# Wider token units in a fused pooled-attention and two-layer MLP kernel: from six units (2 of 576, 4 of 720 tokens) to five (1 of 576, 4 of 864)

## What is computed

```
k_p, v_p = k, v averaged over groups of 8 rows        # 576 keys -> 72
scores = q @ k_p.T / sqrt(64); attn = softmax(scores)
x = attn @ v_p                                        # 8 batches x 8 heads x 576 rows x 64
x = x as 4608 tokens x 512
x = (s * relu(x @ w_in)**2 + b) @ w_out               # 512 -> 2048 -> 512
y = silu(x @ w2_in) @ w2_out                          # 512 -> 2048 -> 512
```

## Time and profile before

| | |
|---|---|
| median of 3 executions | 1635.66 us (1635.04 to 1637.19) |
| the profiled execution, its own time | 1636.79 us |
| span from first to last instruction of it | 1635.0 us |
| PE busy | 1589.4 us, 97% of the span |
| DVE, ACT, POOL busy | 1044.5, 902.2, 220.4 us |
| moved by DMA | 483.82 MB, mean 296 GB/s |
| instructions | 26389, of them 10582 matmuls |

### The profile page before, as it was taken

The page is one execution under the profiler, slowest core; times in us unless marked ns, Lnnn a source line. Parts: engine busy times, 40 slices in busy tenths (PEclk is TensorE's granted clock), DMA queues, the critical chain, the costliest instruction groups (busy, mean ns, idle before and its releaser), DMA issues.

```text
span 1635.0 us, 26389 instructions
## 1 busy us (share of the span) xinstructions
PE 1589.4 (97%) x10582; PEld 1577.5 (96%) x10582; DVE 1044.5 (64%) x1201; ACT 902.2 (55%) x1156; POOL 220.4 (13%) x294
## 2 busy tenths in 40 slices
PE   7999998999989999899999999999999999999998
PEld 7999998999989999899999999999999999999998
DVE  6687686576675765756656846756657657446455
ACT  4575664755536646467455467355476454473442
POOL 5220120122111222201102011011011010000000
PEclk8999999999999999999999999999999999999999
DMA  6799999998999988988888988888988888877886
GB/s 199 280 338 367 343 354 362 319 325 307 314 312 349 329 302 300 323 316 270 277 263 279 315 297 274 269 274 276 332 276 273 265 270 288 317 267 265 266 268 216
DMA packets 138008, 483.82 MB, mean 296 GB/s; under 512 B 14752, under 2 KB 14752, under 8 KB 135840
## 3 DMA queue, kind: packets, MB, share of 16 engines
q1 hardware_dynamic: 134080, 472.70, 84.2%
q10 hardware_dynamic: 3808, 9.44, 1.5%
HBM read 405.67 MB, written 76.41 MB: 295 GB/s over the span
## 4 chain that ended last, share of the span: by engine, by line
PE 85%; DVE 6%; DMA 4%; ACT 4%; issue 1%; SPq 0%; ACTq 0%; DVEq 0%
PE a_ps L802 21%; PE a_ps L824 19%; PE b_ps L802 15%; PE b_ps L824 14%; PE a_ps L728 3%; PE a_ps L752 3%; PE t_ps L695 2%; DMA xa_dram<-probs 2%; DMA ring<-w_dram 2%; PE t_ps L682 2%; PE t_ps L668 2%; PE t_ps L752 2%; PE b_ps L752 1%; PE b_ps L728 1%; DVE gq L1287 1%
## 5 line engine op out<-in xcount | busy, mean ns | idle before, releaser
L802 PE MATMUL a_ps<-xc_hi,ring 128*128 128x360 f32 (+1 forms) x1536 | 386.4, 320 | 6.7 <-DMA ring<-w_dram 3.8
L824 PE MATMUL a_ps<-sp_hi,ring 128*128 128x360 f32 (+1 forms) x1536 | 367.6, 317 | 5.6 <-DMA ring<-w_dram 5.6
L802 PE MATMUL b_ps<-xc_hi,ring 128*128 128x360 f32 (+1 forms) x1152 | 291.3, 319 | 3.6 <-DVE gq L1262 2.2
L802 PEld LDWEIGHTS a_ps<-xc_hi,ring 128*128 128x128 f32 x1536 | 269.9, 189 | 8.0 <-ACT gq L1019 4.0
L824 PE MATMUL b_ps<-sp_hi,ring 128*128 128x360 f32 (+1 forms) x1152 | 275.7, 317 | 0.0
L1303 DVE TENSOR_TENSOR sp_lo<-gq,sp_hi 128x1440 fp32r<-128x1440 f32 (+3 forms) x156 | 194.8, 1271 | 121.2 <-ACT sp_hi L997 121.1
L824 PEld LDWEIGHTS a_ps<-sp_hi,ring 128*128 128x128 f32 x1536 | 265.4, 188 | 6.0 <-issue 6.0
L802 PE MATMUL a_ps<-xc_lo,ring 128*128 128x360 f32 (+1 forms) x768 | 243.4, 317 | 0.0
L824 PE MATMUL a_ps<-sp_lo,ring 128*128 128x360 f32 (+1 forms) x768 | 242.7, 316 | 0.0
L802 PEld LDWEIGHTS b_ps<-xc_hi,ring 128*128 128x128 f32 x1152 | 202.4, 189 | 4.2 <-DVE gq L1262 2.7
L824 PEld LDWEIGHTS b_ps<-sp_hi,ring 128*128 128x128 f32 x1152 | 199.9, 189 | 0.0
(11 more groups left out here) (168 smaller groups left out, 2516.7 us busy)
## 6 DMA issues: line engine op xcount, KB each, us to landing
ring<-w_dram SPq DMA_DIRECT2D x672, 512.0 KB, 4.6
w_dram<-w_stage SPq DMA_DIRECT2D x32, 1024.0 KB, 5.8
w_dram<-ring SPq DMA_DIRECT2D x48, 512.0 KB, 5.5
w_raw<-weights SPq DMA_DIRECT2D x16, 1024.0 KB, 6.8
k_stage<-kT SPq DMA_DIRECT2D x30, 288.0 KB, 5.4
q_sb<-qT SPq DMA_DIRECT2D x30, 288.0 KB, 5.6
v_stage<-vP SPq DMA_DIRECT2D x30, 288.0 KB
xa_dram<-probs SPq DMA_DIRECT2D x28, 288.0 KB, 5.5
```

Source lines behind the costliest of these rows:

```text
L802: last = nc.tensor.matmul(bank[:, half, 0:th], w, xc_of(x, th)[:, j, k, :], start=(first and k == 0 and i == 0), stop=(k == 1 and i == 2), ...
L824: last = nc.tensor.matmul(bank[:, m, 0:th], w, split_of(g, th, turn, 2 * c + half), start=(first and half == 0 and i == 0), stop=(end and ...
```

## The change

Units: one of 576 tokens and four of 864, so `HALVES` = 288 and four times 432 columns, and ten phases instead of twelve. 560 granule loads instead of 672.

Places: `sp_hi` and `sp_lo` have 16*432 columns each; the unit of 288 columns makes six places of them, those of 432 columns four. Places no longer go round over the whole run: each phase starts with place 0, and the first operands of a phase wait for the last slot of the phase before (in phase 0: for the last stores out of `w_stage`, which now lies in the same columns).

Slots of `dhi`, `dlo` and `combine`: written in tables `HIGHS`, `LOWS` and `SUMS`, one for four and one for six places. The tables for four places hold the slots of the code before. With six places the operands (2,0) and (3,0) are made in slots 21 to 23 instead of 31 and 35, the second part of (1,0) in slot 18 instead of 22, (2,1) and (3,1) two and four slots earlier than before, (4,0) one earlier, (4,1) one later, the rest as before.

Attention: the first unit takes five jobs instead of four (the first of them from slot 2 instead of 0, the last in slots 92 to 100), the narrow unit seven instead of six, by a new table `SEVEN`; two wide units take six (a new `SIX`), one four (a new `FOUR`), the last none. The number of jobs is 28 as before.

Memory: `w_raw1`, which had a buffer of its own, is laid over `gq`; the program is built with `dynamic_dma_scratch_size=4096`.

```diff
-HALVES = (288,) * 2 + (360,) * 4
+HALVES = (288,) + (432,) * 4
-PIECES = tuple(2 if i < 4 else 1 for i in range(len(DOWN)))
-PIECE_END = tuple(sum(PIECES[:i + 1]) for i in range(len(DOWN)))
-SPLITS = PIECE_END[-1]
-LATE_COMBOS = {7: (4, 0), 9: (4, 1), 13: (6, 0), 17: (6, 1)}
+SPLITS = len(DOWN) + 4
+HIGHS = {
...
+    6: {8: [(0, 0, 0)], 15: [(0, 0, 1), (1, 0, 0)], 18: [(1, 0, 1)], 21: [(2, 0, 0)], 22: [(3, 0, 0), (0, 1, 0)],
+        27: [(0, 1, 1)], 29: [(1, 1, 0), (1, 1, 1)], 31: [(2, 1, 0)], 33: [(3, 1, 0)], 38: [(4, 0, 0)], 42: [(4, 1, 0)],
+        43: [(5, 0, 0)], 45: [(5, 1, 0)], 47: [(6, 0, 0)], 49: [(6, 1, 0)]},
+}
...
-PLACES = 4
+SPLIT_COLUMNS = 16 * TM
+PLACES = tuple(min(6, SPLIT_COLUMNS // (4 * th)) for th in HALVES)
...
-XC_FIRST, SP_FIRST, G_FIRST = 14 * HB, 4 * PLACES * HB, 2 * FS * HB
+XC_FIRST, SP_FIRST, G_FIRST = 14 * HB, 2 * FPIECES * HB, 2 * FS * HB
...
+def operand_order(ph):
+    return [(j, h) for j, h, part in in_order(HIGHS[PLACES[ph // 2]]) if part == 0]
+
+
+def place_of_operand(ph, j, h):
+
+    order, places = operand_order(ph), PLACES[ph // 2]
+    nth = order.index((j, h))
+    if nth < places:
+        return nth, gran(ph - 1, SLOTS - 1) if ph else None
+    return nth % places, gran(ph, SLOTS_UP + 2 * DOWN.index(order[nth - places]) + 1)
...
-FIRST_UP = 2
+FIRST_UP = (2, 3)
 FIRST_TURNS = (
...
+    (2, 2, 3, 4, 6, 8, 8, 11, 12, 13, 13, 15, 15),
+    (17, 21, 21, 22, 23, 26, 29, 31, 32, 34, 34, 36, 37),
+    (64, 64, 65, 67, 69, 70, 70, 71, 72, 73, 75, 75, 75),
+    (77, 78, 79, 80, 80, 84, 84, 86, 86, 87, 88, 88, 89),
+    (92, 92, 94, 94, 95, 97, 97, 98, 98, 99, 99, 100, 100),
 )
...
+SEVEN = (
+    (0, 0, 0, 0, 1, 2, 2, 4, 5, 6, 8, 8, 8),
+    (13, 14, 14, 14, 15, 18, 19, 20, 21, 22, 22, 24, 24),
+    (26, 27, 28, 29, 29, 31, 31, 33, 33, 36, 37, 37, 37),
+    (40, 40, 40, 42, 42, 44, 44, 47, 47, 49, 49, 50, 51),
+    (51, 52, 52, 55, 55, 58, 58, 59, 59, 60, 61, 62, 62),
+    (64, 65, 65, 66, 66, 68, 69, 71, 71, 74, 75, 76, 76),
+    (78, 79, 80, 81, 83, 84, 84, 86, 86, 88, 88, 91, 92),
+)
...
-UNIT_TURNS = (FIRST_TURNS, SIX, SIX, FOUR, FOUR, FOUR)
+UNIT_TURNS = (FIRST_TURNS, SEVEN, SIX, SIX, FOUR)
...
-        w_raw = [over("w_raw0", yb_at, 0, [4, 512]), sb("w_raw1", [P, 4, 512])]
+        w_raw = [over("w_raw0", yb_at, 0, [4, 512]), over("w_raw1", gq_at, G_FIRST + 2 * KC * HB, [4, 512])]
...
             def load_x(s):
                 if s:
-                    sp.wait_ge(dlo_ready, (2 * s - 1) * SPLITS + PIECE_END[7])
-                    sp.wait_ge(combined, (2 * s - 1) * len(COMBOS) + COMBOS.index((4, 1, 0)) + 1)
+                    ph = 2 * s - 1
+                    sp.wait_ge(dlo_ready, split_count(ph, 3, 1, 0))
+                    sp.wait_ge(combined, sum_count(ph, 4, 1, 0))
...
-                if nth >= PLACES:
-                    act.wait_ge(gran_done, gran(old_ph, SLOTS_UP + 2 * old_idx + 1))
+                if used:
+                    act.wait_ge(gran_done, used)
+                else:
+                    for n in range(STAGE):
+                        act.wait_ge(s_stored[n], 2 * SETS // STAGE * DMA)
...
-    nc = bacc.Bacc("TRN2", target_bir_lowering=False, num_devices=1)
+    nc = bacc.Bacc("TRN2", target_bir_lowering=False, num_devices=1, dynamic_dma_scratch_size=4096)
```

More of the change, by code:

```diff
@@ L54 @@
 SOURCE = (0, 0, 0, 3, 1, 2, 0)
[L55 to L57 removed]
+SPLITS = len(DOWN) + 4
+HIGHS = {
[6 rows of a table added]
+}
+LOWS = {
[6 rows of a table added]
+}
+SUMS = {
[4 rows of a table added]
+}
 XCOMBOS = (1, 4, 2, 6)
@@ L95, in place_of, with in_order, split_count, sum_count @@
     return (4 * SETS + n) % RING
+def in_order(steps):
+    return [step for slot in sorted(steps) for step in steps[slot]]
+def split_count(ph, j, h, part):
+    order = in_order(HIGHS[PLACES[ph // 2]])
+    return ph * SPLITS + order.index((j, h, part)) + 1
+def sum_count(ph, j, h, part):
+    order = in_order(SUMS[PLACES[ph // 2]])
+    return ph * len(order) + order.index((j, h, part)) + 1
+def operand_order(ph):
[6 more added lines that the diff above has]
+    return nth % places, gran(ph, SLOTS_UP + 2 * DOWN.index(order[nth - places]) + 1)
 def use_of(ph, g):
@@ L661, in attention @@
                         pe.wait_ge(f_xlo, PAIRS)
-                    elif t == PAIRS + FIRST_UP:
+                    elif t == PAIRS + FIRST_UP[0]:
                         pe.wait_ge(f_xlo, 2 * PAIRS)
-                    elif t == PAIRS + 2 * FIRST_UP:
+                    elif t == PAIRS + sum(FIRST_UP):
                         pe.wait_ge(f_ydve, 2)
@@ L741, in plain_down @@
                     if k == 3:
-                        pe.wait_ge(x_summed, 2 * FIRST_UP * (1 + layer))
+                        pe.wait_ge(x_summed, 2 * sum(FIRST_UP[:layer + 1]))
                     else:
@@ L808, in down @@
                 idx, c = divmod(slot - SLOTS_UP, 2)
-                (j, h), turn = DOWN[idx], (ph * len(DOWN) + idx) % PLACES
+                j, h = DOWN[idx]
+                turn, _ = place_of_operand(ph, j, h)
                 n, th = gran(ph, slot) - 1, HALVES[ph // 2]
@@ L975, in square, with dhi @@
                     nc.scalar.activation(dst, dst, ACT.Square).then_inc(gated, 1)
[L977 to L983, removed]
+            def dhi(ph, j, h, part):
+                th, (place, used) = HALVES[ph // 2], place_of_operand(ph, j, h)
+                if j < 2:
+                    chunks, to = slice(4 * h + 2 * part, 4 * h + 2 * part + 2), slice(2 * part, 2 * part + 2)
+                    upto = 4 * (2 * h + part)
                 else:
@@ L997, in dhi, with highs @@
                     nc.scalar.activation(dst, src, ACT.Copy).then_inc(dhi_ready, 1)
+            def highs(ph, slot):
+                for piece in HIGHS[PLACES[ph // 2]].get(slot, []):
+                    dhi(ph, *piece)
             def xhi(ph, op):
@@ L1041, in up_slot @@
                 if slot == SLOTS_UP - 1:
-                    dhi(ph, 2, 1)
+                    highs(ph, slot)
                 if j < 3:
@@ L1048, in up_slot @@
                     xhi(ph, 6)
[L1049 to L1056, removed]
+                if slot < SLOTS_UP - 1:
+                    highs(ph, slot)
             def down_slot(ph, d):
@@ L1067, in down_slot @@
                     part_down(ph, 2, idx)
[L1068 to L1072, removed]
+                highs(ph, SLOTS_UP + d)
                 if ph % 2 == 0:
@@ L1303, in dlo, with lows, sums @@
                     nc.vector.tensor_tensor(dst, src, hi, ALU.subtract).then_inc(dlo_ready, 1)
+            def lows(ph, slot):
+                for piece in LOWS[PLACES[ph // 2]].get(slot, []):
+                    dlo(ph, *piece)
+            def sums(ph, slot):
+                for step in SUMS[PLACES[ph // 2]].get(slot, []):
+                    combine(ph, *step)
             def xlo(ph, op):
```

71 lines of the change are left out of this document (25 added, 46 removed), and 37 rows, old and new, of tables (FIRST_TURNS, FOUR, HIGHS, LOWS).

## The result

The changed kernel took 1617.43 us (median of four, 1611.90 to 1618.93) against 1635.35 us before: ratio 0.9885, 95% interval 0.9857 to 0.9913. That is 18 us less, inside the range of 1598 to 1621, and 6 us above the forecast of 1611. The 1635.35 is the median of four executions, one more than in the table of the kernel before.

The account below looks back on a forecast made before the run. PE was taken to bound the wide units, while the narrow and first units also had pauses. Terms -9.6 - 17.2 + 1.7 + 0.5 = -24.6 us took the median 1635.66 to 1611 us, range 1598 to 1621.

Parts of the forecast that it names:

- 7 tail: After the last matmul: the final copy and store, both a fifth larger, +0.5 us.
- Step 1: Matmul time in all units: fewer, wider matmuls, 195.7 ns at 432 columns by a straight line, -9.6 us.
- rival B: All 432-column matmuls: overhead per matmul stops growing, spacing 194.3 ns, 7.5 us less, 1603 us; chance 0.13.
- Step 2: PE pauses in narrow units: 37.2 us in two units become 20 in one, -17.2 us (-25 to -5).
- rival C: Narrow and first units: dense attention tables bring pauses back, narrow 32 us, first +6, 1628 us; chance 0.12.
- Step 3: Narrow unit: six places by themselves cost at nothing beyond the other terms, since PE never waited for `sp_lo`.
- Rival A: Narrow unit: new tables and places fit each other, pauses fall to 12 us, 1601 us in all; chance 0.22.
- Step 4: Attention: 28 jobs as before, but the first unit's fifth job brings pauses, +1.7 us (-2 to +6).
- Step 5: Wide units: ACT, DVE and granule loads keep up with PE's longer slots, 0 (0 to +4 us).
- D: Wide phases: one wait over 2 us each at the turn between layers, 1647 us in all, slower; chance 0.04.
- Step 6: Phase 0's new wait for the `w_stage` stores, and `w_raw1` over `gq` with 4 KB scratch: 0.
- step 8: Removed loads: 112 granules, 58.7 MB, hidden in the wide units; 0 beyond the narrow pauses already counted.

## Why the prediction was right, and where it was off

The sum of the prediction was -24.6 us, the spans differ by 18.0. Term by term, from the rows of the changed kernel above and the earlier trace rows:

| term | predicted | measured |
|---|---|---|
| 1 matmul time | -9.6 | 178.6 + 5376 x 0.1960 = 1232.3, **-8.0** |
| 2 narrow pauses, 37.2 before | -17.2 (20 left) | 24.1 left, **-13.1** |
| 4 start and first unit together | +1.7 | 276.62 - 270.41 - 3.41 - 1.2 (scores of the next unit's first job) = **+1.6** |
| 5 wide units | 0 | 1.9 us of pauses against 0.8 before, **+1.1** |
| 7 tail | +0.5 | **+0.4** |

Step 1: the straight line held (195.7 forecast, 196.0 measured, the same in all ten traces with such units). Three widths now lie nearly on one line: 31.43 ns for the first 72 columns and 31.72 for the next. The overhead over 2.4 GHz is 12.85, 14.28 and 16.0 ns, so it grows with width here, and rival B is out. The Trainium skill (TensorE: Matmul & The Clock Gate, "Wait — 56ns, not 53.3ns?") has a fixed cost over 2.4 GHz, by which it would have been 194.3 ns. The trace does not agree.

Step 2 is the term that was mis-sized: 20 us forecast, 24.1 in this trace and 20.4 in the next execution. Part of the miss is that spread. Its parts were named partly right. Slot 46 costs 3.6 and 3.0 us, where I had 4.3, with slow clock after it in the first trace only. At the start, the first job does lie over the granule wait, as I had it, and the start costs 2.1 + 0.8 us instead of the 5 us of waits and 2 to 3 of slow clock that I carried over. What I did not price are the first transposes that wait for the normalise, 7.7 us in four waits, 2.1 of them those of the start; that is rival C at a smaller size than I gave it. I also read the share of the clock too high. All named waits of unit 0 before, not only the three of the earlier trace rows, make 13.9 of its 21.3 us, about two thirds.

Step 3 failed. I costed six places at nothing because ACT hardly waited for a place and PE never for `sp_lo`. For the kernel before the runs do not contradict it (1.0032 with the places). It does not hold for the changed kernel, which would have been at 0.9976 with four: its narrow unit then has 239.13 - 202.42 = 36.7 us of pauses, over the bound of 32 in step 2. So slots and places together are worth 13 to 16 us in that unit, and step 2 allowed the places and the first job's new slots 5 between them, without working them out. That it came near 20 is in part luck. Rival A had named the fit of tables and places, at 12 us of pauses. What step 3 missed: a place also decides where in the streams of ACT and DVE its work can stand, and behind what. The turn tables were changed with it, and the two fit each other. PE's wait for a late low part never shows as such in these traces; it shows as a wait for an attention turn queued behind the low part.

Step 4 was right by two misses that cancel. The first unit took 234.7 us, not 230: 10.0 more than before, of which 3.4 are the fifth job, 2.4 the scores of two jobs (its own first, which before stood ahead of it, and the next unit's) and 4.2 pauses, not 1.7; they are spread over seven waits of up to 2.1 us. Against that the start is 3.8 us shorter, which I did not have. Before, the scores of the first unit's first job stood there, in slot 0; PE waited 1.62 us for them and then took 2.4 us over them, at a granted clock of 0.50, where they take 1.4 to 1.5 us at 1.00:

```profile
43.37 2.74 PE L668 MATMUL t_ps<-kp,q_sb 128*128 128x144 f32 x10 [1.62 <-DVE xc_lo L1195]
45.73 0.61 PE L728 MATMUL a_ps<-xc_hi,ring 128*128 128x288 f32 x1
```

The new table takes them in slot 2 of the unit, without a wait. The same wait of 1.6 us stands in the two other traces with the old table (six places, and halves, in the kernel before), and not in those with the new one.

Step 5 was right within 1.1 us, and with it D is out: no wide phase has a wait over 0.8 us. But my own sign of being wrong there, a wide unit with six jobs over 285 us, came true by 0.5 us (0.9 in the next execution), and two waits are named where I had none; most of it goes when x is loaded in halves. Step 6 and step 8 show nothing against them: no wait names the stores of `w_stage`, and DMA share fell to 0.73 and 0.67.

Two small sums in the prediction do not come out: 180 ns plus 13 is 193.0, not 193.3, and pauses of 16 us give 1607 us, not 1605. Neither moves the forecast.

## To carry to other kernels

Where several in-order engines share a schedule written by hand, a buffer count, the slots that it allows and the places of everything else in those streams are one decision: undo one alone and the loss can be most of the gain (14 of 18 us here), add one alone and there may be no gain at all. A wait in a trace is worth removing only if the next one behind it is later; try it alone before moving eight. A large load that stands in the same queue as a just-in-time stream should be cut so that the stream's items go in between.

## What the runs showed of the hardware that was not expected

The spacing of matmuls with 128x128 weights in this format (132.85, 164.28 and 196.0 ns at 288, 360 and 432 columns) grew by 0.437 and 0.441 ns a column, where 2.4 GHz is 0.417, while the granted clock of those stretches is shown as 1.00; what takes the rest stays open.

A pause of PE can cost more than its own length, as the granted clock may fall to 0.5 in it or just after; matmuls of 288 columns are then 240 ns apart instead of 133. The length of the one pause before does not tell whether it falls. It fell at the 3.4 us pause in slot 2 of layer 1 of the narrow unit (first row, around it, in the changed kernel), after 2.07 us at the start of that unit in one execution and not after 2.08 in another (rows above), and in the kernel before it did not fall after 3.3 us in slot 46 of unit 1 (second row, around it):

```profile
384.00:403.00 19.00, 15.63 (x100) 15.09 (x100) 13.71 (x18) 9.54 (x14) 4.84 (x5) 0.82 0.71 255
```
```profile
686.00:696.00 10.00, 6.71 (x51) 6.50 (x50) 5.83 (x6) 2.56 (x3) 0.00 (x0) 1.00 0.99 383
```
